# Scores of two heads interleaved on TensorE, the local mask moved to VectorE, and a periodic step table, in a kernel of attention and two MLPs

## The chip, the core and the metric

The kernel runs on one core of a Trainium2 chip. The metric is the device time of one execution in microseconds (us). The engines are TensorE (PE, with its weight loads as PEld), VectorE (DVE), ScalarE (ACT), GpSimd (POOL) and SyncE (SP), which here only issues DMAs. Each engine works through its own list in order; they meet at semaphores.

## The reference

```python
B, H, S, D = 4, 8, 576, 64;  factor = 4
# 1. attention over means of 4 tokens, repeated 4 times
q_d, k_d, v_d = means of q, k, v over groups of 4 tokens      # 144 rows
out_up = repeat(softmax(q_d @ k_d.T / 8) @ v_d, 4)
# 2. local attention: only |i - j| < 4
scores = where(|i - j| < 4, q @ k.T / 8, -1e9)
x = out_up + softmax(scores) @ v                              # 2304 x 512
# 3. first MLP
h = x @ w_in;  x = (h * cos(h)) @ w_out                       # 512 -> 2048 -> 512
# 4. second MLP: RMS norm, gate and value, silu
out = (silu(xn @ w_gate) * (xn @ w_val)) @ w_out2             # 512 -> 1536 -> 512
```

## The kernel before

**Stages.** The 32 heads are taken as 16 pairs, four per batch; a pair's two heads lie on partitions 0 to 63 and 64 to 127 of `qk`. Batch 0 is computed first, by itself, with many PSUM banks (the class `Wide`). Then the first MLP runs in six chunks of 384 tokens, and during the first three chunks the attention of batches 1, 2 and 3 is computed in the gaps (the class `Narrow`, with one bank X and one bank Z for everything). Then come three chunks without attention, and last the second MLP.

**A chunk of the first MLP.** TensorE goes through steps 0 to 18. At step f it does `up(f)` (12 matmuls of 384 columns), then what `attend(…, f, 0)` finds in its table, then the down product of f - 3 (9 matmuls of 512 columns), then what `attend(…, f, 1)` finds. Around `up(f)`, VectorE makes the angle in two instructions (L1047, L1049), ScalarE the sine (L751), VectorE the product (L1055), ScalarE the high part (L684) and VectorE the low part (L964). `up(f)` waits only for the product of f - 3. VectorE and ScalarE have the same two places per f as TensorE has, half 0 before the sine or the low part, half 1 after the product or the sine.

**A pair.** VectorE forms the means (`down_qk`). TensorE puts a mask (three bf16 matmuls against the identity) and then ten 64x64 window products into the score bank (`local`), and two products of 144 columns for the means (`downsampled`). VectorE takes the maximum and subtracts it (`less_local_max`, `down_max`), ScalarE takes the exponentials (`exps`, which needs another activation table than the sine), VectorE sums and inverts (`sum_up`), GpSimd multiplies (`normalise`), TensorE transposes (`transposes`), ScalarE and VectorE copy back, TensorE multiplies with the values (`values`), and ScalarE and VectorE add the result into the chunk's input (`copy_down`, `add_up`). In `Narrow` both heads' local scores use bank X one after the other, and both heads' mean scores bank Z.

**What sets the order.** Written tables. `PE_WHERE` gives for each of the four pairs of a batch the step and half of `scores0`, `local1`, `downsampled1`, `transposes0`, `transposes1` and `values`; `BESIDE_WHERE` does so for VectorE and ScalarE together. GpSimd has no places: it takes value sums and normalisations in order, and in the first batch also splits 16 weight units between the pairs (L517, L519).

Of the kernel before, what the change touches and what calls it, by code (L numbers as in the profile page):

```python
# [14 lines left out]
P = 128  # L15
# [32 lines left out]
WIN = 64  # L48
# [33 lines left out]
def attention_and_two_mlps(nc, qk, vwin, vgrp, w1, wgv, w2, rms_g, const, wsplit, out):  # L82
# [32 lines left out]
    identb = keep("identb", [P, P], BF16)  # L115
    maskb = keep("maskb", [P, 3, WIN], BF16)
# [38 lines left out]
    raw_const = at("raw_const", [P, P + 3 * WIN], F32, xs_at)  # L155
# [49 lines left out]
    class Narrow:  # L205
# [4 lines left out]
        sl, sd = [X[:, 0:TP * WIN]] * 2, [Z[0:QT, 0:2 * SD]] * 2  # L210
# [17 lines left out]
    down_scores = sem("down_scores")  # L228
    lmax_ready = sem("lmax_ready")
# [107 lines left out]
    def hold(eng, semaphore, value):  # L337
# [3 lines left out]
        if not isinstance(value, int):  # L341
# [5 lines left out]
    PE_STEPS = ("scores0", "local1", "downsampled1", "transposes0", "transposes1", "values")  # L347
    PE_WHERE = (((1, 0), (2, 0), (3, 0), (4, 0), (4, 1), (5, 0)),
# [3 lines left out]


    BESIDE_STEPS = ("down_qk", "less_max0", "exps", "copy_pt0", "copy_pt1", "copy_down")
    BESIDE_WHERE = (((-1, 1), (0, 0), (1, 1), (2, 1), (3, 1), (4, 1)),
# [3 lines left out]

    def steps_at(names, where, place):  # L360
        return [(name, j) for j in range(PAIRS) for name, at_ in zip(names, where[j]) if at_ == place]
# [247 lines left out]
    def act_program(act):  # L609
# [19 lines left out]
        def exps(kind, b, j, s):  # L629

            if kind is Narrow and s == 0:
# [54 lines left out]
        def attend(c, f, half):  # L686

            for what, j in steps_at(BESIDE_STEPS, BESIDE_WHERE, (f, half)):
# [170 lines left out]
    def dve_program(dve):  # L859
# [6 lines left out]
        v.tensor_copy(identb[:, :], raw_const[:, 0:P]).then_inc(setup_dve, 1)  # L866
        v.tensor_copy(maskb[:, :, :].rearrange("p a b -> p (a b)"), raw_const[:, P:P + 3 * WIN]).then_inc(setup_dve, 1)
# [23 lines left out]
        def less_local_max(kind, b, j, s):  # L891
# [3 lines left out]
            sl = kind.sl[s].rearrange("p (t k) -> p t k", k=WIN)  # L895
            dve.wait_ge(local_scores, u + 1)
            v.tensor_reduce(lmax[:, s, :], sl, axis=AX.X, op=ALU.max).then_inc(lmax_ready, 1)
            dve.wait_ge(lmax_ready, u + 1)
# [37 lines left out]

        down_qk(Wide, 0, 0)
# [28 lines left out]
        def attend(c, f, half):  # L966

            for what, j in steps_at(BESIDE_STEPS, BESIDE_WHERE, (f, half)):
                if what == "down_qk":
                    down_qk(Narrow, c + 1, j)  # L970
                elif what == "less_max0":
                    less_max(Narrow, c + 1, j, 0)
                elif what == "exps":
                    less_local_max(Narrow, c + 1, j, 1)
                    sum_up(Narrow, c + 1, j, 0)
                    down_max(Narrow, c + 1, j, 1)
# [5 lines left out]
                elif what == "copy_down":  # L982
# [180 lines left out]
    def pe_program(pe):  # L1163
        t_ = nc.tensor

        def local(kind, b, j, s):
# [3 lines left out]
            q, k = (kind.qk[j][64 * s:64 * s + 64, a, :] for a in range(2))  # L1170
            if kind is Narrow:
                if s == 0:
                    pe.wait_ge(x_ready, n)
                else:
# [328 lines left out]
```

## Time and profile before

| | |
|---|---|
| median of three runs | 973.09 us (971.92 to 973.64) |
| the profiled execution's own time | 974.04 us |
| its span | 972.3 us |
| TensorE busy | 951.9 us, 98% |
| VectorE busy | 591.2 us, 61% |
| ScalarE, GpSimd busy | 411.0 us (42%), 308.9 us (32%) |
| second chunk, from the first up matmul to that of the next chunk | 152.66 to 246.19, 93.53 us |
| in it, busy TensorE, VectorE, ScalarE, GpSimd | 93.03, 68.73, 47.40, 26.12 us |

The busy figures are averages over stages with different limits: batch 0 (up to about 55 us) is not bound by TensorE, the rest is. The third chunk takes 93.8 us (246.19 to 340.00). In a timeline, a row merges equal instructions (x20); two matmul records stand for one float32 matmul of the attention.

### The profile page before, as it was taken

The numbers are of one execution on the slowest core, as the hardware profiler recorded it, in microseconds if no ns is written. First come the engines' busy times: TensorE is split into PE (matmuls) and PEld (weight loads), VectorE is DVE, ScalarE is ACT, GpSimd is POOL, SyncE is SP. The second block draws the span as 40 slices with busy tenths as digits, with TensorE's granted clock in tenths as the row PEclk, the third lists the DMA queues.
The fourth block names the chain that finished last, engine by engine and source line by source line (L and its number), as shares of the span: only waits on it lengthen the run. The fifth ranks groups of instructions, "written<-read, shape, count | busy, mean of one in ns | idle before, by whom it ended". The sixth has DMA issues, their size and how long they took to land.

```text
span 972.3 us, 17493 instructions
## 1 busy us (share of the span) xinstructions
PE 951.9 (98%) x6104; PEld 848.5 (87%) x6104; DVE 591.2 (61%) x1225; ACT 411.0 (42%) x889; POOL 308.9 (32%) x366
## 2 busy tenths in 40 slices
PE   7899999999999999999999999999999999999998
PEld 5678888888888899999989988899899899999997
DVE  6668777776876675675768554445644456544344
ACT  4435445544644454454544433334422234433232
POOL 5948873221422165486474220011200002000000
PEclk9999999999999999999999999999999999999999
DMA  9622211111111134354345665555565555575631
GB/s 290 219 71 99 79 54 54 54 53 54 53 55 53 50 128 150 130 195 169 140 161 185 261 210 148 152 157 159 146 217 151 152 161 162 154 227 162 163 98 65
DMA packets 66173, 132.31 MB, mean 136 GB/s; under 512 B 7088, under 2 KB 7216, under 8 KB 66096
## 3 DMA queue, kind: packets, MB, share of 16 engines
q1 hardware_dynamic: 66096, 131.27, 42.8%
q8 instruction: 50, 0.82, 0.3%
q14 instruction: 27, 0.22, 0.1%
HBM read 104.50 MB, written 26.74 MB: 135 GB/s over the span
## 4 chain that ended last, share of the span: by engine, by line
PE 91%; POOL 3%; DVE 2%; issue 1%; ACT 1%; DMA 1%; SPq 0%; POOLq 0%; ACTq 0%; DVEq 0%
PE ps L1268 28%; PE ps L1270 27%; PE ps L1269 27%; POOL W L519 2%; PE ps L1187 1%; PE ps L1204 1%; PE ps L1342 1%; PE ps L1245 1%; PE ps L1221 1%; PE ps L1237 1%; DMA qk<-qk 1%; PE ps L1224 1%; DVE xs L960 0%; POOL vg_more L493 0%; POOL prob L505 0%
## 5 line engine op out<-in xcount | busy, mean ns | idle before, releaser
L1268 PE MATMUL ps<-xo,wu 128*128 128x384 f32 x504 | 168.7, 335 | 1.5 <-DVE gate_a L1090 1.5
L1269 PE MATMUL ps<-xo,wu 128*128 128x384 f32 x504 | 169.9, 337 | 0.0
L1270 PE MATMUL ps<-xo,wu 128*128 128x384 f32 x504 | 169.4, 336 | 0.0
L1268 PE MATMUL ps<-xs,W 128*128 128x384 f32 x384 | 134.6, 350 | 0.9 <-DVE xs L960 0.9
L1270 PE MATMUL ps<-xs,W 128*128 128x384 f32 x384 | 130.5, 340 | 0.0
L1269 PE MATMUL ps<-xs,W 128*128 128x384 f32 x384 | 130.1, 339 | 0.0
L1268 PE MATMUL ps<-W,ring 128*128 128x512 f32 x288 | 116.4, 404 | 0.1
L1270 PE MATMUL ps<-W,ring 128*128 128x512 f32 x288 | 113.4, 394 | 0.0
L1269 PE MATMUL ps<-W,ring 128*128 128x512 f32 x288 | 113.2, 393 | 0.0
L751 ACT ACTIVATE ub<-ub,consts 128x384 f32<-128x384 f32 x96 | 59.1, 616 | 104.9 <-DVE ub L1049 104.2
L1268 PEld LDWEIGHTS ps<-xo,wu 128*128 128x128 f32 x504 | 94.7, 188 | 8.2 <-DVE gate_a L1090 1.8
L1269 PEld LDWEIGHTS ps<-xo,wu 128*128 128x128 f32 x504 | 94.6, 188 | 6.7
L1270 PEld LDWEIGHTS ps<-xo,wu 128*128 128x128 f32 x504 | 94.7, 188 | 0.0
L1270 PE MATMUL ps<-wo,ring 128*128 128x512 f32 x216 | 85.7, 397 | 0.0
L1269 PE MATMUL ps<-wo,ring 128*128 128x512 f32 x216 | 85.4, 395 | 0.0
L1268 PE MATMUL ps<-wo,ring 128*128 128x512 f32 x216 | 85.3, 395 | 0.1
L1047 DVE TENSOR_SCALAR ub<-ps 128x384 f32<-128x384 f32 x96 | 53.0, 552 | 49.3 <-PE ps L1270 49.2
L1095 DVE TENSOR_TENSOR val_b<-val_b,ps 128x384 f32<-128x384 f32 x36 | 20.0, 555 | 98.8 <-ACT val_b L798 98.7
L1268 PEld LDWEIGHTS ps<-xs,W 128*128 128x128 f32 x384 | 73.1, 190 | 6.3 <-issue 1.7
L1269 PEld LDWEIGHTS ps<-xs,W 128*128 128x128 f32 x384 | 73.2, 191 | 1.9
L964 DVE TENSOR_TENSOR ring<-ub,ring 128x384 fp32r<-128x384 f32 x96 | 67.1, 699 | 10.9 <-ACT ring L684 10.6
L1270 PEld LDWEIGHTS ps<-xs,W 128*128 128x128 f32 x384 | 73.1, 190 | 0.0
(132 smaller groups left out, 1730.4 us busy)
## 6 DMA issues: line engine op xcount, KB each, us to landing
wu<-wsplit SPq DMA_DIRECT2D x252, 256.0 KB, 2.8
wsplit<-wp SPq DMA_DIRECT2D x84, 256.0 KB, 2.0
W_raw<-w SPq DMA_DIRECT2D x8, 1024.0 KB, 14.6
qk<-qk SPq DMA_DIRECT2D x14, 576.0 KB, 4.2
gv<-wgv SPq DMA_DIRECT2D x12, 512.0 KB, 3.7
vw<-vwin SPq DMA_DIRECT2D x14, 384.0 KB, 3.2
out<-XY SPq DMA_DIRECT2D x18, 256.0 KB, 3.6
vg<-vgrp SPq DMA_DIRECT2D x26, 144.0 KB
```

What stands on the lines that cost most here:

```text
L519: g.tensor_tensor(lo, raw, hi.bitcast(F32), ALU.subtract).then_inc(unit_ready, 1)
L751: a.activation(v, v, ACT.Sin, scale=-2.0 * math.pi, bias=consts[:, 1:2]).then_inc(cos_ready, 1)
L964: v.tensor_tensor(ring[:, f % 3, 1, :], ub[:, f % 2, :], ring[:, f % 3, 0, :].bitcast(F32), ALU.subtract).then_inc(glo_ready, 1)
L1047: v.tensor_scalar(w, HB[f % NH], 0.25, MAGIC, ALU.add, ALU.add).then_inc(angle0, 1)
L1095: v.tensor_tensor(vb[:, :], vb[:, :], CB, ALU.add).then_inc(vb_ready, 1)
L1187: ins = t_.matmul(sl[64 * half:64 * half + 64, t * WIN:t * WIN + WIN], q[:, Q0[w]:Q0[w] + WIN], k[:, K0[w]:K0[w] + WIN], start=False, stop ...
L1204: ins = t_.matmul(kind.sd[s][:, t * SD:t * SD + SD], q[:, t * QT:t * QT + QT], k, start=True, stop=True)
L1221: t_.transpose(kind.pt[:, k * P:k * P + P], kind.prob[j][:, s, 2 * k:2 * k + 2, :].rearrange("p a b -> p (a b)"), ident[:, :])
L1224: ins = t_.transpose(kind.ptd[:, k * SD + t * QT:k * SD + t * QT + QT], kind.probd[j][0:QT, s, t, k * QT:k * QT + QT], ident[0:QT, 0:QT])
L1268: t_.matmul(dst, a_lo, b_hi, start=first, stop=False, skip_group_check=True)
L1269: t_.matmul(dst, a_hi, b_lo, start=False, stop=False, skip_group_check=True)
L1270: return t_.matmul(dst, a_hi, b_hi, start=False, stop=last, skip_group_check=True)
```

## The change

Three things change together. The mask is no longer accumulated by TensorE: it is stored for all five tiles (`maskb` of 5 x 64 columns, `identb` goes, and the constant that is loaded grows from 320 to 448 columns), and VectorE adds it in an instruction of its own. In the chunks, both heads' scores are computed side by side, alternating head by head, one head in bank X and the other in bank Z (local scores X and Z, mean scores the same two once the masked sums are out). And the tables become one row that repeats every four steps from step 4j + 1 for pair j: TensorE's `local` at 0, `downsampled` at 1, `transposes0` at 2 (half 1), `transposes1` at 3, `values` at 3 (half 1). The means are formed two steps ahead. VectorE and ScalarE have tables of their own.

```diff
-    PE_STEPS = ("scores0", "local1", "downsampled1", "transposes0", "transposes1", "values")
-    PE_WHERE = (((1, 0), (2, 0), (3, 0), (4, 0), (4, 1), (5, 0)),
...
+    PE_STEPS = ("local", "downsampled", "transposes0", "transposes1", "values")
+    PE_AT = ((0, 0), (1, 0), (2, 1), (3, 0), (3, 1))
+    DVE_STEPS = ("down_qk", "diff", "down_max", "sum0", "sum1", "copy_pt0", "copy_pt1", "add_up")
+    DVE_AT = ((-2, 1), (0, 0), (1, 0), (1, 1), (2, 0), (2, 1), (3, 0), (3, 1))
+    ACT_STEPS = ("exps", "copy_pt0", "copy_pt1", "copy_down")
+    ACT_AT = ((1, 1), (2, 1), (3, 0), (3, 1))
...
             dve.wait_ge(local_scores, u + 1)
-            v.tensor_reduce(lmax[:, s, :], sl, axis=AX.X, op=ALU.max).then_inc(lmax_ready, 1)
-            dve.wait_ge(lmax_ready, u + 1)
             free = n - kind.lag
             if not (isinstance(free, int) and free < 0):
                 dve.wait_ge(pv_done, free + 1)
-
+            v.tensor_tensor(p, sl, maskb[:, :, :], ALU.add).then_inc(masked_ready, 1)
             v.memset(kind.prob[j][:, s, TP, :], 0.0)
-            v.tensor_tensor(kind.prob[j][:, s, 0:TP, :], sl, lmax[:, s, :].unsqueeze(2).to_broadcast([P, TP, WIN]), ALU.subtract).then_inc(diff_ready, 1)
+            dve.wait_ge(masked_ready, u + 1)
+            v.tensor_reduce(lmax[:, s, :], p, axis=AX.X, op=ALU.max).then_inc(lmax_ready, 1)
+            dve.wait_ge(lmax_ready, u + 1)
+            v.tensor_tensor(p, p, lmax[:, s, :].unsqueeze(2).to_broadcast([P, TP, WIN]), ALU.subtract).then_inc(diff_ready, 1)
...
-            t_.matmul(sl[:, 0:WIN], identb[:, :], maskb[:, 0, :], start=True, stop=False, skip_group_check=True)
...
+        def local_both(kind, b, j):
+
+            n = PAIRS * b + j
+            pe.wait_ge(x_ready, n)
+            pe.wait_ge(kind.qk_in[j], 16 * loads(kind, b, j))
+            for w in range(NW):
+                for s in range(2):
+                    ins = local_window(kind, j, s, w)
+            ins.then_inc(local_scores, 2)
+
+        def downsampled_both(kind, b, j):
+
+            n = PAIRS * b + j
+            pe.wait_ge(qkd_ready, n + 1)
+            pe.wait_ge(masked_ready, 2 * n + 2)
+            for t in range(2):
+                for s in range(2):
+                    ins = downsampled_tile(kind, j, s, t)
+            ins.then_inc(down_scores, 2)
```

VectorE, the first pair of a chunk, from the chunk's first product (L1055) to the inverse of the first head's sums. `ub` is the angle and then the product, `ring` the low part, `prob` the local scores of the pair. Before:

```order
L1055 SCALAR_TENSOR_TENSOR ub<-ps,ub 128x384
L1047 TENSOR_SCALAR ub<-ps 128x384
L1049 SCALAR_TENSOR_TENSOR ub<-ub,ps 128x384
L964 TENSOR_TENSOR ring<-ub,ring 128x384
L1055 SCALAR_TENSOR_TENSOR ub<-ps,ub 128x384
L897 TENSOR_REDUCE lmax<-ps 128x5
L903 MEMSET prob_81 128x64
L904 TENSOR_TENSOR prob_81<-ps,lmax 128x320
L923 TENSOR_REDUCE sums<-prob_81 128x5
L926 TENSOR_SCALAR sums<-sums 128x7
L930 RECIPROCAL recip<-sums 128x7
```

After the change (its line numbers are those of the changed file: L894 is the new addition, L1054 the product, L960 the low part, L905 the maximum of the mean scores):

```order
L1054 SCALAR_TENSOR_TENSOR ub<-ps,ub 128x384
L1046 TENSOR_SCALAR ub<-ps 128x384
L1048 SCALAR_TENSOR_TENSOR ub<-ub,ps 128x384
L894 TENSOR_TENSOR prob_80<-ps,maskb 128x320
L895 MEMSET prob_80 128x64
L897 TENSOR_REDUCE lmax<-prob_80 128x5
L899 TENSOR_TENSOR prob_80<-prob_80,lmax 128x320
L894 TENSOR_TENSOR prob_80<-ps,maskb 128x320
L895 MEMSET prob_80 128x64
L897 TENSOR_REDUCE lmax<-prob_80 128x5
L899 TENSOR_TENSOR prob_80<-prob_80,lmax 128x320
L960 TENSOR_TENSOR ring<-ub,ring 128x384
```

The first head's maximum and difference stood ahead of the first product at f = 0, and one head's sums followed in f = 1; now both heads' additions, maxima and differences stand together in f = 1, and the sums come one step later.

TensorE, the second head of a chunk's first pair, before (a float32 row counts one per matmul, not per record):

```order
L1181 MATMUL ps<-maskb,identb 128x64
L1182 MATMUL ps<-maskb,identb 128x192
L1184 MATMUL ps<-maskb,identb 128x64
L1187 MATMUL ps<-qk_77 64x64 x10
L1268 MATMUL ps<-xs,W_49 128x384
```

After, in place of two such groups and of two groups of L1204 with x2, each pair has these two rows, an `up` apart, and its transposes stand half a step behind the third `up`:

```order
L1169 MATMUL ps<-qk_76 64x64 x20
...
L1175 MATMUL ps<-qkd_82 72x144 x4
...
L1226 MATMUL ps<-ident,prob_80 128x128 x3
L1229 MATMUL ps<-ident,probd_81 72x72 x4
```

Three insertions of scores per pair have become two, and no mask stands among them.

## Rows read from the trace of the kernel before

**Rows 1.** The page: busy time of each engine, its share of the span.

```profile
PE 951.9 (98%) x6104; PEld 848.5 (87%) x6104; DVE 591.2 (61%) x1225; ACT 411.0 (42%) x889; POOL 308.9 (32%) x366
```

**Rows 2.** Timeline of PE: start, duration, engine, line, operation, tiles, records.

```profile
203.54 0.20 PE L1181 MATMUL ps<-maskb,identb 128*128 128x64 bf16 x1
...
203.78 0.80 PE L1187 MATMUL ps<-qk 64*64 64x64 f32 x20
204.51 0.45 PE L1268 MATMUL ps<-xs,W 128*128 128x384 f32 x1
204.80 0.34 PE L1269 MATMUL ps<-xs,W 128*128 128x384 f32 x1
204.97 0.35 PE L1270 MATMUL ps<-xs,W 128*128 128x384 f32 x1
...
206.56 0.34 PE L1270 MATMUL ps<-xs,W 128*128 128x384 f32 x1
206.82 0.71 PE L1204 MATMUL ps<-qkd 64*72 64x144 f32 x4
207.46 0.50 PE L1268 MATMUL ps<-W,ring 128*128 128x512 f32 x1
207.80 0.39 PE L1269 MATMUL ps<-W,ring 128*128 128x512 f32 x1
208.03 0.39 PE L1270 MATMUL ps<-W,ring 128*128 128x512 f32 x1
```

**Rows 3.** Timeline of PE, the products with the values of one pair.

```profile
146.96 0.71 PE L1237 MATMUL ps<-probd,vd 72*64 72x144 f32 x8
147.60 0.91 PE L1245 MATMUL ps<-prob,vw 64*64 64x58 f32 x40
```

**Rows 4.** Timeline, start of the second chunk: PE's first up, then DVE.

```profile
152.66 0.33 PE L1268 MATMUL ps<-xs,W 128*128 128x384 f32 x1
...
157.05 0.55 DVE L1047 TENSOR_SCALAR ub<-ps 128x384 f32<-128x384 f32 x1
157.63 0.55 DVE L1049 SCALAR_TENSOR_TENSOR ub<-ub,ps 128x384 f32<-128x384 f32 x1
158.10 0.49 DVE L897 TENSOR_REDUCE lmax<-ps 128x5 f32<-128x320 f32 x1
...
158.70 0.43 DVE L904 TENSOR_TENSOR prob<-ps,lmax 128x320 f32<-128x320 f32 x1
159.04 0.44 DVE L910 TENSOR_REDUCE dmax<-ps 72x2 f32<-72x288 f32 x1
```

**Rows 5.** Timeline: ACT's sine and table load, then POOL's end of a normalisation.

```profile
161.68 0.62 ACT L751 ACTIVATE ub<-ub,consts 128x384 f32<-128x384 f32 x1 [0.53 <-DVE ub L1049]
162.31 1.28 ACT L624 ACT_TABLE_LOAD   x1
...
166.93 0.66 POOL L508 TENSOR_TENSOR probd<-probd,recip 72x288 f32<-72x288 f32 x1 [0.18 <-POOL prob L505]
```

**Rows 6.** Groups of instructions by line on PE: busy, mean ns, idle before.

```profile
L1204 PE MATMUL ps<-qkd 64*72 64x144 f32 x128 | 26.8, 338 | 0.8 <-ACT probd L624 0.8
```

**Rows 7.** Timeline of POOL in the first chunk.

```profile
75.96 1.24 POOL L517 TENSOR_TENSOR W<-W_raw,ones 128x512 fp32r<-128x512 f32 x1
...
89.17 0.72 POOL L493 TENSOR_TENSOR vg<-vg 72x256 f32<-72x256 f32 x1
...
94.31 0.72 POOL L505 TENSOR_TENSOR prob<-prob,recip 128x320 f32<-128x320 f32 x1
```

**Rows 8.** Timeline of POOL in batch 0: two of its normalisations.

```profile
15.01 0.72 POOL L505 TENSOR_TENSOR prob<-prob,recip 128x320 f32<-128x320 f32 x1 [1.54 <-DVE recip L930]
...
47.66 0.66 POOL L508 TENSOR_TENSOR probd<-probd,recip 72x288 f32<-72x288 f32 x1
```

**Rows 9.** Timeline of DVE in the first chunk, while POOL splits weights.

```profile
85.55 1.27 DVE L964 TENSOR_TENSOR ring<-ub,ring 128x384 fp32r<-128x384 f32 x1
```

**Rows 10.** DMA issues of the page: KB of each, median us to landing.

```profile
qk<-qk SPq DMA_DIRECT2D x14, 576.0 KB, 4.2
```

More of the change, by code:

```diff
@@ L342, in hold @@
             eng.sem_inc(passed, 1)
-    PE_STEPS = ("scores0", "local1", "downsampled1", "transposes0", "transposes1", "values")
-    PE_WHERE = (((1, 0), (2, 0), (3, 0), (4, 0), (4, 1), (5, 0)),
[3 rows of a table removed]
-    BESIDE_STEPS = ("down_qk", "less_max0", "exps", "copy_pt0", "copy_pt1", "copy_down")
-    BESIDE_WHERE = (((-1, 1), (0, 0), (1, 1), (2, 1), (3, 1), (4, 1)),
[3 rows of a table removed]
+    PE_STEPS = ("local", "downsampled", "transposes0", "transposes1", "values")
[4 more added lines that the diff above has]
+    ACT_AT = ((1, 1), (2, 1), (3, 0), (3, 1))
     def steps_at(names, where, place):
-        return [(name, j) for j in range(PAIRS) for name, at_ in zip(names, where[j]) if at_ == place]
+        return [(name, j) for j in range(PAIRS) for name, (step, half) in zip(names, where) if (4 * j + 1 + step, half) == place]
     def x_arrived(eng, c, k):
@@ L686, in attend @@
         def attend(c, f, half):
-            for what, j in steps_at(BESIDE_STEPS, BESIDE_WHERE, (f, half)):
+            for what, j in steps_at(ACT_STEPS, ACT_AT, (f, half)):
                 if what == "exps":
@@ L1164, in pe_program, with local_window, downsampled_tile @@
         t_ = nc.tensor
-        def local(kind, b, j, s):
+        def local_window(kind, j, s, w):
+            q, k = (kind.qk[j][64 * s:64 * s + 64, a, :] for a in range(2))
+            half, t = w % 2, w // 2
+            return t_.matmul(kind.sl[s][64 * half:64 * half + 64, t * WIN:t * WIN + WIN], q[:, Q0[w]:Q0[w] + WIN], k[:, K0[w]:K0[w] + WIN],
+                             start=True, stop=True)
+        def downsampled_tile(kind, j, s, t):
+            q, k = (kind.qkd[j][64 * s:64 * s + 64, a, :] for a in range(2))
+            return t_.matmul(kind.sd[s][:, t * SD:t * SD + SD], q[:, t * QT:t * QT + QT], k, start=True, stop=True)
@@ L1168, in local, with scores @@
+        def scores(kind, b, j, s):
             n = PAIRS * b + j
             u = 2 * n + s
[L1170 to L1174, printed above, removed]
-                    pe.wait_ge(diff_ready, u)
-            elif u > 1:
-                pe.wait_ge(diff_ready, u - 1)
+            if u > 1:
+                pe.wait_ge(masked_ready, u - 1)
             if s == 0:
@@ L1196, in downsampled @@
                 pe.wait_ge(qkd_ready, n + 1)
-            if kind is Narrow:
-                if s == 1:
-                    pe.wait_ge(exp_down, u)
-            elif u > 1:
+            if u > 1:
                 pe.wait_ge(exp_down, u - 1)
-            q, k = (kind.qkd[j][64 * s:64 * s + 64, a, :] for a in range(2))
             for t in range(2):
-                ins = t_.matmul(kind.sd[s][:, t * SD:t * SD + SD], q[:, t * QT:t * QT + QT], k, start=True, stop=True)
+                ins = downsampled_tile(kind, j, s, t)
@@ L1291, in attend @@
         def attend(b, step, half):
-            for what, j in steps_at(PE_STEPS, PE_WHERE, (step, half)):
-                if what == "scores0":
-                    scores(Narrow, b, j, 0)
-                elif what == "local1":
-                    local(Narrow, b, j, 1)
-                elif what == "downsampled1":
-                    downsampled(Narrow, b, j, 1)
+            for what, j in steps_at(PE_STEPS, PE_AT, (step, half)):
+                if what == "local":
+                    local_both(Narrow, b, j)
+                elif what == "downsampled":
+                    downsampled_both(Narrow, b, j)
                 elif what == "transposes0":
```

57 lines of the change are left out of this document (25 added, 32 removed), and 6 rows, old and new, of tables (BESIDE_WHERE, PE_WHERE).

## The prediction

> **What bounds the kernel now.** I read the page first. TensorE is busy in 98% of the span, VectorE in 61% [rows 1]. Then the timelines of the chunks with attention: there TensorE's matmuls follow one another, and its only idle time that the grouped view puts down to another engine in the attention's score matmuls is 0.8 us in all, before the mean scores [rows 6]. So from the first chunk on, TensorE time taken out is time gained, as long as nobody else gets late. The other engines are late by little: in a chunk's first pair VectorE takes up its first angle only 4.39 us after TensorE's first up matmul (157.05 against 152.66) [rows 4]. Batch 0, ahead of the chunks, is another stage: from 15 us to 48 us GpSimd works almost without a break, with normalisations at both ends [rows 8].
>
> **What TensorE saves.** A full-size matmul starts 0.17 (384 columns) or 0.23 us (512) after the one before it; an up is 12 x 0.175 = 2.10, a down 9 x 0.23 = 2.07. The second head's masks and windows cost 204.80 - 203.54 - 0.17 = 1.09: 0.24 of masks, 0.73 of windows, 0.12 of return to full size. Its mean scores cost 207.80 - 206.56 - 0.17 - 0.23 = 0.84, of which 0.09 is the way into the small tiles. The first head has both in one insertion, 1.09 + 0.64 = 1.73 [rows 2]. Sum for a pair: 3.66.
>
> How much two heads side by side cost isn't in the trace, so I bound it. Window products with 20 records take 0.80, the value products with 40 records, which alternate in both halves of the array's rows and columns, 0.91; the mean scores take 0.71 for 4 records in whole-width tiles one after the other, the mean's values 0.71 for 8 records that alternate between two column halves [rows 2, 3]. So one bound is "two heads for the price of one", the other "no overlap". I take the first, since the value rows are the nearest. Then a pair costs 0.09 + 0.73 + 0.12 = 0.94 for windows and 0.84 for means, 1.78 together, and 3.66 - 1.78 = 1.88 is saved. Times 12 pairs: **-22.6 us**. Without overlap 0.6 + 0.5 = 1.1 us per pair are missing from it, 13 us in all.
>
> **What arrives late instead: a chunk's first pair.** I write the step times down from the first up matmul (0). TensorE: up(0) and up(1) to 4.2, windows to 5.14, up(2) to 7.24; there it wants the mean scores, which now wait for both heads' masked sums, since they go into the same banks. VectorE starts its first angle at 4.39, the second instruction 0.58 later, and ScalarE's sine follows 0.59 behind that. A VectorE instruction of this size gives way to an independent one after 0.47; a maximum of 320 columns and the subtraction behind it take 0.60 and 0.34 [rows 4]. f = 0: angle 4.39 and 4.97, sine 5.56, product 6.20. f = 1: angle 6.68 and 7.26, first addition 7.73. The addition has no row of its own; the nearest is the subtraction of the same 320 columns out of PSUM, 0.43 [rows 4], and 0.08 to the instruction that needs it. So addition, maximum, subtraction are 0.51 + 0.57 + 0.34 = 1.42 per head, the second addition starts at 9.15 and is done at 9.6. TensorE has waited **2.4 us**.
>
> From there VectorE goes on: maximum and subtraction of the second head to 10.57, low part and product to 11.5, angle of f = 2 at 11.5 and 12.1, sine at 12.7. From a sine to the end of the first head's normalisation the trace has 161.68 to 167.59, 5.91 us, of which 1.28 is the load of the exponential's table [rows 5]. So the transposes can begin at 18.6. TensorE, from 9.6, has mean scores, up(3), down(0) to do, 0.84 + 2.10 + 2.07, and stands at 14.6: **4.0 us** of hole. Before, the first transposes stood behind up(4), and each head's scores went their own way.
>
> The first chunk starts with TensorE slow (below), and VectorE is not behind there; only the second hole counts, with 0.15 of the first. Sum over three chunks: 2 x 6.4 + 4.15 = 16.9, less the 0.8 that stood there before: **+16.1**.
>
> **The other nine first transposes.** Counted from the third up's end, TensorE comes to them after 0.84 + 2.07 + 2.10 + 2.07 = 7.08. VectorE sees that end 0.2 late, needs 0.58 + 0.59 for the angle, and the chain of 5.91 follows: 7.28, plus 0.05 of semaphore: a hole of 0.25 for six pairs, 1.5 us. In the first chunk GpSimd splits five units behind each pair: 75.96 to 89.17 is 13.2, to the next normalisation 5.1 more [rows 7]; with two normalisations of 1.5 (0.72, 0.66 and their gaps) [rows 5, 7] is 21.3, and it begins about 0.6 after the transposes; a pair's four steps take TensorE 4 x 4.17 + 1.78 + 2.9 (transposes, values) = 21.4. Hole about 0.6 with the semaphore, three times: 1.8. Together **+3.3**.
>
> **The last pair's second transposes** stand directly behind the first, without a product between (there is no up(16)). GpSimd normalises the second head 0.5 behind the first, 1.5 long; TensorE is there after 0.63. Hole 1.35, three times: **+4.0**.
>
> **Batch 0.** Masks leave TensorE there too, but GpSimd sets the pace, and what counts is when its row of work starts. Both additions of the first pair lie ahead of it. The first is covered by the wait for the second pair's load; the second is not: +0.5. The subtraction now reads SBUF twice, as L964 does, which took 1.27 while GpSimd worked, where others of 384 columns take 0.55 [rows 4, 9]: 0 to 0.7 more. The constant's load grows by 64 KB ahead of the first `qk`, 0.2 to 0.5 when 576 KB take 4.2 [rows 10]. **+1.1**, between 0.6 and 1.5. The later pairs have more room than they lose.
>
> That a subtraction with two SBUF inputs waits for GpSimd is also what the Trainium skill says (SBUF — State Buffer, "Who interferes with whom": a VectorE instruction with two SBUF inputs contends with a GpSimd instruction that reads SBUF). By a reading in which GpSimd never matters, the sum would be 0.6 lower; the row decides for the rule.
>
> **Nothing for** the means two steps ahead (that step of VectorE holds only an angle, a product and copies besides, and the `qk` load, 4.2 us [rows 10], has a step and a half), the memset, the shorter setup. If that cover were gone, the mean's 1.3 us would stand in front of an angle, and the chain behind would be late by as much.
>
> **Sum.** -22.6 + 16.1 + 3.3 + 4.0 + 1.1 = +1.9. The profiled execution took 974.04, so 975.9 on its scale. The median of the runs lies 0.95 lower, so I say 975.0. Its own range is 972 to 979: the chain enters 12 holes, so 0.2 us less in it are 2.4 us less in all, and a lock of 0.3 per pair is 3.6 more. VectorE has no cover for such a lock: in the step with both heads' masks it works 0.58 + 0.47 + 2 x 1.42 + 0.95 = 4.84, and TensorE ends the next up 0.94 + 2.07 + 2.10 = 5.11 after the last. A measurement here tells about 0.2% (1.95 us) from nothing.
>
> **Rivals.**
> (a) *The holes are smaller than I make them, and the kernel is faster.* The point is the chain behind a chunk's first pair. If half of the 16.1 goes, the result is 967; if all 23.4 stayed out, 952. For it: what I chain are starts with waits in them. Against: every link is a row, and the order on VectorE and ScalarE is fixed. It decides from 4 us less hole in all on. 0.17.
> (b) *The clock falls in the holes.* The granted clock reads 1.00 throughout, but ahead of 62.8 us the same up matmuls follow one another by 0.32 instead of 0.17 us, behind a stage in which TensorE did small attention products and waited, so the lower of the levels, 1.2 GHz, exists here. A fall in a hole of 4.0 us would cost what that start costs, some 13 matmuls x 0.15 = 1.9, in each of three chunks: 981. Against: holes are short beside the busy stretches. 0.12. The Trainium skill's page TensorE: Matmul & The Clock Gate, Part 1, says that an array left idle goes back to half rate, and speaks against this change; its own sum would be this rival's.
> (c) *The heads don't overlap.* 13 us are missing, but a TensorE that is slower also waits less (each transposes' hole shrinks by what stands ahead of it, about 5 us in all): 983. Against it stand the value rows. 0.08.
> (d) *My sum*, 0.63, about a third of it within 0.2% of before.
>
> **Numbers.** Likeliest 975.0. The range takes in (d), the nearer part of (a) and (b): 969 to 982. Faster by over 0.2% is (a) with a rest of (d): 0.18. Within: 0.27. Slower: (b), (c) and the rest of (d): 0.55.
>
> **What would show it.** Right: no L1181 to L1184; 40 window records in 0.8 to 0.9 us; TensorE idle about 2.4 us before the mean scores and 4 us before the transposes of each first pair in the second and third chunk, with GpSimd's normalisation as releaser; a chunk about as long as before (93.5 us). Wrong: a chunk of 88 us or less (then the chain was shorter), 40 records in 1.5 us (no overlap), or up matmuls 0.32 us apart behind a hole (the clock).

## The result, and the profile after

| | before | after |
|---|---|---|
| median of 4 runs each | 973.37 us | 987.82 us (986.53 to 991.8) |
| ratio, 95% interval | | 1.0162 (1.0145 to 1.018) |
| span of the profiled execution | 972.3 us | 984.7 us |
| start of the first, second, third, fourth chunk | 54.96, 152.66, 246.19, 339.54 us | 56.98, 157.43, 254.77, 352.00 us |

The change makes the kernel 1.6% slower. I had forecast 975.0 us within 969 to 982: the sign was right, the time is 12.8 us off and outside my range. Behind the start of the fourth chunk the two executions are the same again; the 12.4 us between the spans arise before. (The third chunk of the kernel before ends at 339.54 us, so it took 93.35 us, not the 93.8 given ahead.) One execution of `before_shifted` below took 1316.6 us at a mean granted clock of 0.67, a slow state, and enters no comparison.

The page of after: the busy line (it answers to [rows 1]), the instruction queues, the chain that ended last. PE is busy 16 us less in a longer span.

```profile
PE 936.1 (95%) x6008; PEld 835.0 (85%) x6008; DVE 603.8 (61%) x1256; ACT 409.7 (42%) x889; POOL 310.5 (32%) x366
...
q14 instruction: 38, 0.31, 0.1%
...
PE 77%; DVE 10%; issue 6%; ACT 4%; POOL 2%; DMA 0%; DVEq 0%; ACTq 0%; SPq 0%; POOLq 0%
```

The windows of after, one row a chunk with attention; behind the busy times of the engines stands the granted clock:

```profile
56.98:157.43 100.45, 91.35 (x779) 77.39 (x777) 75.84 (x189) 45.96 (x100) 61.34 (x64) 0.97 0.22 73
157.43:254.77 97.34, 89.28 (x777) 76.08 (x776) 72.24 (x183) 46.84 (x104) 25.11 (x37) 0.96 0.18 54
254.77:352.00 97.23, 88.57 (x777) 75.39 (x776) 72.05 (x183) 46.84 (x104) 25.35 (x37) 0.96 0.16 50
```

The second chunk took 93.53 us before. TensorE now has 89.28 us of work in it instead of 93.03 and is 3.8 us slower through it: 8 us of holes (stretches in which TensorE waits), and a clock that reads 1.00 no longer.

PE's timeline at the second chunk's first pair (the place of [rows 2]):

```profile
161.71 0.81 PE L1169 MATMUL ps<-qk 64*64 64x64 f32 x40
162.45 0.44 PE L1273 MATMUL ps<-xs,W 128*128 128x384 f32 x1
...
169.95 1.24 PE L1175 MATMUL ps<-qkd 64*72 64x144 f32 x8 [5.15 <-DVE prob L894]
171.12 0.69 PE L1273 MATMUL ps<-xs,W 128*128 128x384 f32 x1
171.61 0.52 PE L1274 MATMUL ps<-xs,W 128*128 128x384 f32 x1
171.93 0.52 PE L1275 MATMUL ps<-xs,W 128*128 128x384 f32 x1
...
178.84 0.55 PE L1226 MATMUL ps<-ident,prob 128*128 128x128 f32 x3 [1.15 <-POOL probd L502]
```

Three readings. The 40 windows take 162.45 - 161.71 = 0.74 us: the heads overlap. The mean scores wait 5.15 us, where I had 2.4. And behind that wait the same up matmuls follow one another by 0.32 instead of 0.17 us. The windows of the same stretch show the granted clock (the third number from the end) fall to 0.50, which is 1.2 of 2.4 GHz, within the 5 us without a matmul:

```profile
162.00:166.00 4.00, 2.81 (x48) 2.42 (x40) 2.37 (x3) 0.30 (x1) 3.34 (x5) 1.00 0.01 2
166.00:170.00 4.00, 0.05 (x2) 0.08 (x3) 3.59 (x10) 1.45 (x3) 1.23 (x2) 0.87 0.48 135
170.00:174.00 4.00, 4.00 (x17) 3.63 (x18) 3.86 (x11) 1.63 (x3) 0.00 (x0) 0.50 0.37 99
174.00:178.00 4.00, 3.70 (x14) 2.89 (x12) 2.67 (x7) 3.97 (x13) 0.72 (x1) 0.78 0.23 85
```

Why 5.15? VectorE's timeline at the start of the same chunk (the place of [rows 4]):

```profile
158.46 2.13 DVE L1067 COPY XY<-ps 128x512 f32 x3 [1.67 <-ACT ub L768]
163.26 1.35 DVE L869 TENSOR_REDUCE qkd<-qk 128x288 f32<-128x1152 f32 x1 [2.67 <-issue]
164.53 0.55 DVE L1046 TENSOR_SCALAR ub<-ps 128x384 f32<-128x384 f32 x1
```

Between the last instruction of the loop over the chunks (L1067) and its first (L869) VectorE stands still for 2.67 us and waits for nothing that the profile names ("issue"). The first angle comes 7.10 us after the first up, not 4.39 [rows 4]. In the full list of VectorE's instructions the next one comes 3.02 and 2.93 us after the compare-and-branch that jumps back; before the change it was 0.31 and 0.28 (measured from start to start). The page's q14 row (instruction packets, 8 KB each) has 38 packets where the page of before has 27.

### The profile page after: what moved, and what is told of

The parts are those of the page before. It is cut to its first block, busy times and chain, and to the rows that moved or that the text cites. A ratio compares the mean times of both kernels' runs of the same rounds, so it can differ in the third digit from the quotient of the medians.

```text
span 984.7 us, 17345 instructions
## 1 busy us (share of the span) xinstructions
PE 936.1 (95%) x6008; PEld 835.0 (85%) x6008; DVE 603.8 (61%) x1256; ACT 409.7 (42%) x889; POOL 310.5 (32%) x366
## 4 chain that ended last, share of the span: by engine, by line
PE 77%; DVE 10%; issue 6%; ACT 4%; POOL 2%; DMA 0%; DVEq 0%; ACTq 0%; SPq 0%; POOLq 0%
PE ps L1273 24%; PE ps L1275 23%; PE ps L1274 23%; DVE ub L1046 2%; ACT L618 2%; PE ps L1250 1%; PE ps L1226 1%; DVE prob L894 1%; PE ps L1242 1%; DVE lmax L897 1%; PE ps L1345 1%; DVE ub L1048 1%; POOL prob L499 1%; ACT probd L618 1%; DVE ring L960 1%
## 5 line engine op out<-in xcount | busy, mean ns | idle before, releaser
L960 DVE TENSOR_TENSOR ring<-ub,ring 128x384 fp32r<-128x384 f32 x96 | 65.1, 678 | 9.5 <-ACT ring L678 9.5
```

Source lines behind the costliest of these rows:

```text
L960: v.tensor_tensor(ring[:, f % 3, 1, :], ub[:, f % 2, :], ring[:, f % 3, 0, :].bitcast(F32), ALU.subtract).then_inc(glo_ready, 1)
```

## The experiments

**Is the pause a load of code?** Counted in the traces from 0, VectorE's loop body ran from its instruction 139 to 443 before and from 147 to 459 after (eight additions a chunk). The Trainium skill, Advanced Engine Details and Errata, "ISA Cache", says that an engine holds code in two lines of 256 instructions. By that, a body that touches a third line can't stay resident. I had not weighed that rule. The next two kernels move the body and change no work, by one edit that stands ahead of everything (56 in after_shifted, 16 in before_shifted):

```diff
         v = nc.vector
+        for n in range(56):
+            v.memset(X[:, n:n + 1], 0.0)
         v.memset(consts[:, 0:1], MAGIC).then_inc(zeroed, 1)
```

after_shifted. 

> The changed kernel with 56 one-column memsets on VectorE ahead of everything (they write scratch columns of PSUM that nobody reads, at a time when VectorE waits for a constant). They only shift the later code of VectorE by 56 instructions. Theory (instruction fetch): the 2.9 us between the jump back at the end of VectorE's loop over the chunks and its next instruction are a load of code, which depends on how many blocks the loop body touches; the body (313 instructions in the trace) starts at the 147th instruction and ends at the 459th, and if blocks are 128 instructions with a border near 450 it touches four of them; shifted by 56 it touches three. Then the jump takes 0.3 us as before the change, the hole ahead of the first mean scores falls from 5.2 to about 2.6 us in the second and third chunk, and the time falls by at least 5.2 us to 982.6; to 978 if the clock then stays up too. Rival (the pause is a wait of the new order, not a fetch): no change, 987.8.

Measured: 982.86 us, ratio to before 1.0102 (1.0084 to 1.012). The body stands at 203 to 515. Page and timeline:

```profile
q14 instruction: 28, 0.23, 0.1%
```

```profile
158.87 2.13 DVE L1069 COPY XY<-ps 128x512 f32 x3 [1.67 <-ACT ub L768]
161.00 1.35 DVE L871 TENSOR_REDUCE qkd<-qk 128x288 f32<-128x1152 f32 x1
```

No pause, and the time is the 982.6 expected; the wait of the mean scores is 2.48 us, my 2.4. From 159 to 164 us, around the jump, q14 moved one packet here and three in the kernel after the change.

before_shifted. 

> The kernel before with 16 such memsets on VectorE, nothing else. Theory (fetch): its loop body (305 instructions, from the 139th to the 443rd) now ends at the 459th and touches a fourth block; the jump back takes about 3 us instead of 0.3, twice; VectorE's first product is 2.7 us later, and TensorE, which had about 1 us to spare there, waits 1.5 to 2 us per chunk: 976 to 977.5 instead of 973.4. Rival (the pause belongs to the new order): 973.4, jump of 0.3.

Measured: 978.04 us, 1.0052 (1.0034 to 1.007), body at 155 to 459; the second and third chunk take 95.88 and 95.81 us instead of 93.53 and 93.35.

```profile
q14 instruction: 38, 0.31, 0.1%
```

```profile
152.15 2.13 DVE L1070 COPY XY<-ps 128x512 f32 x3 [1.68 <-ACT ub L774]
156.78 1.35 DVE L878 TENSOR_REDUCE qkd<-qk 128x288 f32<-128x1152 f32 x1 [2.49 <-issue]
```

Its time is 0.5 us above the 976 to 977.5 expected; its pauses are 2.85 and 2.79 us, and TensorE waits 1.83 and 1.76 us behind them. So the load of code (the "fetch" of the expectations) holds on both sides: the same work gets the pause or loses it when the body is moved. The pause doesn't belong to the new order. A border lies between the instructions 444 and 459; the kernel before ended at most 15 short of it. How long the blocks of code are is not settled: three blocks of 128, as my expectation had it, fit all these runs as well as two of 256.

**Which part of the change costs?**

masks_only (the addition alone, in the kernel before):

```diff
+            v.tensor_tensor(p, sl, maskb[:, :, :], ALU.add).then_inc(masked_ready, 1)
...
-                    pe.wait_ge(diff_ready, u)
+                    pe.wait_ge(masked_ready, u)
...
-            t_.matmul(sl[:, 0:WIN], identb[:, :], maskb[:, 0, :], start=True, stop=False, skip_group_check=True)
```

> The kernel before (its tables, its scores head by head) with the mask added by VectorE alone. TensorE saves 24 x 0.24 = 5.8 us of mask matmuls. Batch 0 costs 2.0 more (as measured in the changed kernel). Theory (fetch): eight additions lengthen the loop body to 313 instructions as in the changed kernel, so the jump pause of 3 us is there as well and costs 1.5 to 2 us twice: about 973. Rival (the pause comes from the new order): no pause, 969.6. If the additions themselves make VectorE late in the first pair, 1 us per chunk more in either case.

Measured: 978.33 us, 1.0053 (1.0035 to 1.0071). The pause is there (2.87 and 2.79 us; body again 147 to 459, 38 packets), and behind it 2.0 us of idle TensorE and up matmuls 0.32 us apart. The pause was predicted; the time is 5.3 us above the 973 expected, and the next kernel shows that most of this is neither pause nor clock.

masks_only_shifted (the same with the 56 memsets). 

> masks_only with 56 memsets ahead, so that the loop body of VectorE no longer touches a further block. masks_only measured 978.3: chunks of 95.7 us with a pause of 2.9 us at the jump, 2 us of TensorE idle before the first mean scores and a granted clock of 0.98. Theory (pause plus the clock's fall are what it costs; the additions themselves are hidden): the hole and the fall go, each of the second and third chunk gets 2.2 + 1.3 us shorter, to 92.2; 978.3 - 7 = 971 to 972, slightly under the kernel before, since TensorE saves 5.8 us and batch 0 costs 2.5. Rival (the additions themselves make VectorE late): 974 to 976.

Measured: 974.42 us, 1.0013 (1.0003 to 1.0022): 3.9 us less than masks_only, the pause gone and the clock at 1.00, but not the 971 to 972 of the theory; it is the rival's 974 to 976 (the additions make VectorE late). TensorE still waits 1.05 and 1.43 us before the mean scores of the first pairs, and the first chunk begins at 58.16 us, 3.2 later than before. So what the masks save on TensorE (5.8 us) is spent on VectorE's later chain and in batch 0.

interleave_only (the new order, masks left on TensorE: the diff of the change without its lines on `maskb` and `masked_ready`). 

> The changed kernel (both heads side by side, new table) with the masks still accumulated by TensorE and no addition on VectorE. TensorE has 12 x 0.48 = 5.8 us more. VectorE's chain to the second head's release of its bank is as long (maximum, difference, maximum, difference), behind it 0.9 us shorter. The loop body is back at 305 instructions. Theory (fetch): no pause at the jump; hole ahead of the first mean scores 1.9 us, ahead of the first transposes about 2.6; the 0.32 us holes of the later pairs vanish; batch 0 as before: 981 if the clock falls behind the holes as in the changed kernel, 976 if it stays up. Rival (the pause comes from the new order): 5 to 6 us more than that.

Measured: 977.87 us, 1.0043 (1.003 to 1.0057); body 139 to 443, no pause, as expected. The waits of the second chunk's first pair:

```profile
161.43 0.71 PE L1180 MATMUL ps<-qkd 64*72 64x144 f32 x8 [2.14 <-DVE prob L898]
...
169.26 0.55 PE L1234 MATMUL ps<-ident,prob 128*128 128x128 f32 x3 [2.73 <-POOL probd L502]
```

So the order alone costs its first pair's two holes, and each half of the change by itself is no faster than before. The half that crosses the border is the masks.

The halves don't add up. With the pause gone from both, the masks cost 0.13%, the order 0.43%, and the two together (after_shifted) 1.02%. The starts of the chunks say where: the first begins at 54.75 us in interleave_only and at 57.73 in after_shifted, the second at 151.59 and 157.84, and behind that after_shifted is the faster one (190.62 us against 191.75 for two chunks). So the additions cost 2 to 3 us in batch 0 (the kernel after the change, without memsets ahead, begins its first chunk at 56.98) and 3.3 in the first chunk, the two stretches in which GpSimd also splits weights. Under the old order they cost as much in batch 0 (57.43 in masks_only) but nothing in the first chunk, which takes 95.00 us there.

**What does the clock cost?** fill_holes:

```diff
+    FILL = {"downsampled": 12, "transposes0": 14}
...
+                if j == 0 and what in FILL:
+                    pe.wait_ge(g_done, F1 * (b - 1) + step + 2)
+                    for _ in range(FILL[what]):
+                        t_.matmul(HB[(step + 1) % NH], w_part(2 * step, 0)[:, 0:P], xs[:, 0, 0, :], start=True, stop=True, skip_group_check=True)
```

> after_shifted with matmuls whose results nobody reads, put into a chunk's two first-pair waits of TensorE: 12 of 384 columns before the first mean scores, 14 before the first transposes (they write the bank of the next up matmul, which overwrites it). The computation is as before. TensorE waits as long as before but is busy meanwhile. Theory (the granted clock falls because TensorE was idle, and costs 1 to 2 us after each hole): no stretch of the attention chunks is granted less than 0.9; the second and third chunk get 1.5 to 2 us shorter, the first loses 1.3 us more than it gains in the first hole (12 x 0.17 = 2.1 us in a hole of 0.8) and gains 1.4 behind the second: 979 to 980 against the 982.9 of after_shifted. Rival (the clock falls for another reason, for instance power or the small score matmuls): clock as in after_shifted, 983 to 984.

Measured: 983.15 us, 1.0096 (1.008 to 1.0113): nothing gained, where I had expected 979 to 980. Behind the filled holes the matmuls keep their distance of 0.17 us, but the time goes into the next wait (the first transposes stand until GpSimd has normalised, whether TensorE was slow before or not), and the clock now fell at the last pairs of the first and second chunk.

fill_all (the waits over 0.5 us of those chunks filled in this way). 

> after_shifted with matmuls whose results nobody reads in every wait of TensorE over 0.5 us of the attention chunks: before the first mean scores 4 in the first chunk and 15 in the other two, before the first transposes 22 and 20, before those of pairs 2 and 3 a few (3 and 9 in the first chunk, 1 later), between the last pair's transposes 7. The computation is as before. Theory (the clock falls behind idle time, and costs real time only where nothing later is waited for anyway): the falls of after_shifted that count are those behind the first chunk's first transposes (1.5), its third pair (1.35) and the second chunk's last pair (1.5), 4.4 us together: no stretch under 0.95, 978 to 979. Rival (the rest of the difference is holes, the clock costs nothing net): 982.9, or some tenths more for fillings that are too long.

Measured: 981.13 us, 1.0092 (1.0075 to 1.0109). Its windows, a row a chunk:

```profile
57.85:157.50 99.65, 96.35 (x824) 83.47 (x822) 76.25 (x189) 45.87 (x100) 61.64 (x64) 1.00 0.22 74
157.50:252.07 94.57, 94.21 (x821) 81.32 (x820) 71.67 (x183) 46.84 (x104) 25.77 (x37) 1.00 0.18 55
252.07:346.47 94.40, 94.06 (x822) 81.25 (x821) 71.77 (x183) 46.83 (x104) 25.43 (x37) 1.00 0.17 51
```

and those of after_shifted:

```profile
57.73:157.84 100.11, 91.26 (x778) 77.81 (x777) 75.32 (x189) 45.94 (x100) 61.51 (x64) 0.97 0.22 73
157.84:254.00 96.16, 89.81 (x777) 76.31 (x776) 71.88 (x183) 46.84 (x104) 25.47 (x37) 0.96 0.17 54
254.00:348.46 94.46, 88.18 (x777) 75.23 (x776) 71.77 (x183) 46.83 (x104) 25.34 (x37) 0.98 0.17 51
```

The clock stays at 1.00, though three holes of 0.7 to 1.3 us are left in the first chunk: with TensorE busy in the others the falls are gone, so they come from idleness. What they cost is small and depends on the place. The third chunk of after_shifted had a clock of 0.98 and is as long as with 1.00, because its fall lay ahead of a hole. The second had one more, behind the last pair's transposes, where nothing waits afterwards: nine down matmuls took 3.81 us there instead of 2.24, and the chunk is 96.16 instead of 94.46. The gain of 1.7 us in the medians is within the two intervals, so only the traces show it; the 4.4 us that I expected did not come.

**Can the holes be taken out?** pairwise:

```diff
+            for s in range(2):
+                sl = kind.sl[s].rearrange("p (t k) -> p t k", k=WIN)
+                v.tensor_tensor(kind.prob[j][:, s, 0:TP, :], sl, maskb[:, :, :], ALU.add).then_inc(masked_ready, 1)
...
+            v.tensor_reduce(lmax[:, :, :], p, axis=AX.X, op=ALU.max).then_inc(lmax_ready, 2)
...
+            v.tensor_tensor(p, p, lmax[:, :, :].unsqueeze(3).to_broadcast([P, 2, TP, WIN]), ALU.subtract).then_inc(diff_ready, 2)
```

> after_shifted, VectorE takes both heads of a pair together in the chunks: both additions first, then one maximum and one subtraction over both heads (640 columns). The second bank is released after two additions (1.0 us) instead of addition, maximum, subtraction, addition (1.93), and the whole takes about 2.45 instead of 2.9. Theory (the hole ahead of the first mean scores is VectorE's chain up to the second addition): that hole falls from 2.7 to 1.8, the one ahead of the transposes by another 0.4, and the 0.3 us holes of the later pairs by 0.2 to 0.3: 3 x 1.9 - 0.5 = about -5 us, 978; if the clock stays up then, 975. Rival (the holes come from something later, the table load or GpSimd): 982.9.

Measured: 986.18 us, 1.013 (1.0113 to 1.0147), *slower* than after_shifted (1.0102) by some 3 us. Its trace is of the slowest of its four executions (988.75 us):

```profile
165.88 0.71 PE L1192 MATMUL ps<-qkd 64*72 64x144 f32 x8 [1.43 <-DVE prob L910]
...
175.57 0.69 PE L1243 MATMUL ps<-ident,prob 128*128 128x128 f32 x2 [4.61 <-POOL probd L502]
```

The first hole shrank from 2.48 to 1.43 as expected. But VectorE's chain as a whole is only 0.25 us shorter (both heads in 2.65 instead of 2.90), so the time went into the next hole (2.23 to 4.61; between the two holes TensorE needed 5.08 us instead of 6.66, since no slow clock fell there, and that too is waited for). And behind this single long one the clock fell where it counts: the up behind it took 3.99 us instead of 2.17. The expectation added up holes of which the second is the first one's remainder.

own_first_row and own_row_pairwise give the first pair its own places:

```diff
+    PE_FIRST = ((0, 0), (1, 0), (3, 0), (3, 1), (4, 0))
+    DVE_FIRST = ((-2, 1), (-1, 1), (0, 0), (0, 1), (1, 0), (1, 1), (2, 0), (3, 0))
+    ACT_FIRST = ((0, 1), (1, 1), (2, 0), (3, 0))
```

> after_shifted with a row of its own for each batch's first pair: VectorE adds, takes maxima and subtracts after the first product (f = 0, half 1) instead of ahead of the second, ScalarE takes the exponentials and VectorE the rest one half step or more earlier than the periodic row says, and TensorE comes to the first transposes half a step later (after the fourth up), to the second after the next down, and to the values after the fifth up. Theory (the loss is the VectorE chain behind a chunk's first pair): the addition of the second head ends 1.1 us earlier (hole 1.6), the exponentials come a whole step earlier, so no hole ahead of the transposes: per chunk -1.1, -2.9 (-3.8 in the first) and with them most of the clock's fall (-1.7): about 982.9 - 17 = 966, 3 us more if the product of f = 1, which is now late by 2.8 us, makes an up wait. Rival (the gaps only move to the next place, the values or the second pair's scores): 978 or more.

> Both of the last two edits together. If they add up: own_first_row minus 3 to 4 us (the first hole falls to 0.6, three small holes of later pairs by 0.2 to 0.3 each in three chunks), so about 962 to 963. Rival (once the first pair is in order nothing waits for VectorE's chain): the time of own_first_row.

Measured: 978.54 us, 1.0051 (1.0034 to 1.0068), and 976.68 us, 1.0046 (1.0031 to 1.006). Chunks of 94.42 and 92.87, and of 93.99 and 92.11 us. Against after_shifted that is 4.3 us where some 17 were expected (the time is the rival's, 978 or more), and 6.2 where some 20 were. The trace of the second shows holes that are left or new: in each of these chunks 1.7 us between the first pair's values and the second's windows (VectorE has to empty the banks), and 2.05 and 1.44 us before the first down (the profile names no releaser; in VectorE's order the low part of f = 0 stands behind the mean maxima).

own_row_mended moves these places (OWN1 is the second pair), the next two build on it:

```diff
-    DVE_FIRST = ((-2, 1), (-1, 1), (0, 0), (0, 1), (1, 0), (1, 1), (2, 0), (3, 0))
+    DVE_FIRST = ((-1, 0), (-1, 1), (0, 1), (0, 1), (1, 0), (1, 1), (2, 0), (3, 0))
+    OWN1 = {PE_AT: ((0, 1), (1, 0), (2, 1), (3, 0), (3, 1)), DVE_AT: DVE_AT, ACT_AT: ACT_AT}
```

> own_row_pairwise with three places moved, each after a wait that its trace shows. (1) The second pair's windows go behind the next down product instead of directly behind the first pair's values: TensorE waited 1.75 us there for VectorE to empty the banks. (2) The first pair's mean maxima stand behind the product of f = 1 instead of ahead of the low part of f = 0: the first down waited 1.6 us for that low part. (3) The means of the first pair are formed after the chunk's first angle instead of ahead of it (1.27 us of VectorE at the chunk's start, 0.69 of it now beside the sine). Theory (in the attention chunks all that is left to gain is waits for VectorE's order): each chunk 3 to 3.5 us shorter, about 89 in the second and third, and hardly a hole in which the clock could fall: 976.7 - 10 to 12 = 965 to 967. Rival (each wait taken away appears at the next place, as in pairwise): 973 or more.

> own_row_mended, with the masks of batch 0 alone back on TensorE (they are multiplied with every second bf16 half of the float32 identity, and VectorE takes maximum and difference from PSUM there as before). Theory (batch 0 is bound by VectorE and GpSimd, not by TensorE, and VectorE's additions and the longer constant cost 2 to 2.7 us there): the first chunk begins at about 55.2 instead of 57.7, the rest is the same: 2.5 us faster than own_row_mended, about 963. Rival (batch 0 is late for another reason, e.g. the code or the load of the constant): no change.

> masks_in_batch0_on_pe, with the last pair's second transposes of TensorE behind the next down product and its values behind the one after. Theory (the hole of 1.33 us between the last pair's transposes is the wait for the second normalisation): it goes, but the values come 0.7 to 2 us later with one down product (2.04 us) instead of two behind them, and copying, adding and splitting take about 2.5 us until the next chunk's first up: from 1 us faster to 2 us slower in all; likeliest within 1 us. Rival (the split isn't ready in time): 1 to 1.5 us per chunk slower.

Measured: 975.32 us, 1.0026 (1.0015 to 1.0038); 977.33 us, 1.0037 (1.0023 to 1.0051); 970.2 us, 0.9972 (0.9957 to 0.9988). The first was a miss (965 to 967 expected, its rival 973 or more), for a reason that its trace gives: the second pair's windows now come half a step later and its transposes didn't, so they wait 1.82 us, with a clock's fall behind them. (That trace is of its slowest execution, 980.42 us; the other seven lie between 974.89 and 976.84.) The masks of batch 0 back on TensorE let the first chunk begin at 56.0 and 55.2 us (the traces of the second and third kernel) instead of 57.5, but no gain shows in the medians (the second kernel's is even 2.0 us higher; its runs lie between 971.9 and 978.27). Spreading the last pair is the first version under the kernel before. It gained 7.1 us where at most 1 was expected: the three holes of 1.3 us between the last pair's transposes are gone, 3.9 us, and its trace has two falls of the clock instead of four; how much of the rest these account for was not tried.

half_step_rows carries that on to every pair. It still has the joint subtraction of pairwise, the masks of batch 0 on TensorE and the idle memsets ahead:

```diff
+    PE_HALF = ((0, 1), (1, 0), (3, 0), (3, 1), (4, 0))
+    PE_LAST = ((0, 1), (1, 0), (2, 1), (3, 1), (4, 1))
...
+            rows = (PE_FIRST, PE_HALF, PE_HALF, PE_LAST)
```

> last_pair_spread, and now every pair but the first has its windows behind the down product (half 1) and every pair but the last its first transposes behind the next up instead of ahead of it, the second behind the down product after it and the values behind the up after that, so that no two steps of a pair stand side by side. VectorE's and ScalarE's tables are as before. In last_pair_spread TensorE waits 2.0 us before the second pair's first transposes in each chunk, and the clock falls behind it (1.5 us). Theory (the waits are differences of a few us between VectorE's chain and TensorE's distance, and a step more of distance takes them away): the hole of the second pair goes, with it the fall; chunks of 88 to 88.5 us instead of 90 to 91.4, 970.2 - 3 x 2.5 = about 962.5. Rival (VectorE, which waits in its order for the later transposes and values, now makes an up late): no gain or a loss, 970 or more.

> half_step_rows, with the first pair's mean maxima on VectorE between the low part of f = 0 and the product of f = 1, where VectorE waits 0.7 us for the sine, instead of behind that product. The hole before the first pair's first transposes was 1.15 us. Theory: that chain is 0.5 to 0.6 us earlier, the hole 0.6: 1.5 us faster than half_step_rows. Rival (the hole is set by the sine and the exponentials of ScalarE, which come in the same order): no difference.

Measured: 966.21 us, 0.9937 (0.992 to 0.9953), and 966.73 us, 0.9941 (0.9925 to 0.9958). half_step_rows is 0.6% faster than the kernel before. Its windows:

```profile
55.19:155.64 100.45, 91.98 (x778) 77.33 (x777) 74.29 (x180) 45.80 (x100) 62.75 (x65) 0.98 0.22 73
155.64:244.81 89.17, 86.79 (x777) 73.80 (x777) 70.17 (x176) 46.58 (x105) 25.08 (x37) 1.00 0.19 59
244.81:333.71 88.90, 86.52 (x778) 73.81 (x777) 70.15 (x176) 46.61 (x105) 25.35 (x37) 1.00 0.16 50
```

The second and third chunk lose 4.4 us each against before. The first does not (100.45 us against 97.70), and there lies most of the 3.7 us by which the expectation was missed; this trace is of the slowest of four executions (968.35 us, the others 965.43 to 966.23). Moving the mean maxima did nothing: the first pair's hole stays at 1.0 us.

## Why the prediction was wrong

Between the profiled spans 12.4 us were measured and 1.9 predicted. That the sign came out right is mostly luck: 10.5 of the 12.4 us are not in my sum. By its own steps (a hole is counted here to the next start that was possible, which is 0.15 to 0.2 us more than the bracket of the timeline for the transposes):

- *What TensorE saves (-22.6).* Right: 0.74 us for 40 windows and 0.64 for the eight mean scores, to the next start. "The heads don't overlap" is out.
- *"VectorE starts its first angle at 4.39".* This is the step that failed. I took the start of the chunk over from the trace of before, as if only instructions could move it. It is 7.10, because the longer code no longer stays loaded across the jump back. The same chain from there is right: with the pause gone the hole is 2.48 for my 2.4, and from the sine to the end of the normalisation it is 5.91 us in both. Price: 2.7 us in two chunks, 5.4, half of the 10.5; the shift gave back 5.0 in the medians.
- *Rival (b), the clock.* It came true in all three chunks, with 0.12 on it. Its size was wrong in both directions: in the second and third chunk the fall behind 5.2 us of idleness lengthened TensorE's work (in the second by 2.7 us) and cost nothing, since the transposes behind it waited for the chain anyway (their hole is 1.3 and 2.2, where I had 4.0); in the first chunk it counts twice, 1.1 + 0.4 behind the first transposes and 1.4 at the last pair, together 3.0.
- *The other first transposes (+3.3).* In the later chunks 0.30 to 0.34 for my 0.25 (no row showed the 0.2 and 0.05 us that I added there for seeing an end and for a semaphore). In the first chunk 0.6, 1.9 and 1.5 for my 0.6 each, 2.2 more. GpSimd's queue, on which I had put it, was not behind (it waited for VectorE's inverse, 1.65, 1.04 and 0.72 us). VectorE was slow itself beside GpSimd's splitting; the new subtraction and the low part, which both read SBUF twice:

```profile
110.54 1.43 DVE L899 TENSOR_TENSOR prob<-prob,lmax 128x320 f32<-128x320 f32 x1
...
112.93 0.49 DVE L899 TENSOR_TENSOR prob<-prob,lmax 128x320 f32<-128x320 f32 x1
113.34 1.63 DVE L960 TENSOR_TENSOR ring<-ub,ring 128x384 fp32r<-128x384 f32 x1
```

  GpSimd beside it:

```profile
110.33 1.29 POOL L513 TENSOR_TENSOR W<-W_raw,W 128x512 fp32r<-128x512 f32 x1
...
112.95 1.60 POOL L513 TENSOR_TENSOR W<-W_raw,W 128x512 fp32r<-128x512 f32 x1
```

  The subtraction that starts behind GpSimd's instruction takes 1.43 us, the one that starts 0.02 ahead of it 0.49, and then GpSimd's takes 1.60 instead of about 1.28. interleave_only, whose subtraction reads PSUM, has no hole over 0.3 us before the first transposes of the other three pairs of this chunk; since it has no additions either, it doesn't tell the two apart, and the lock's share of the 2.2 us is read from the rows only.

  I knew this lock [rows 9] and priced it in batch 0 alone, and as 0.3 a pair in the range.
- *The last pair (+4.0).* 1.5 for 1.35 per chunk, right.
- *Batch 0 (+1.1).* The last split before the first chunk starts at 59.48 for 58.50, so 1.0: right. Part of it is made good because the up matmuls are at 0.17 us from 59.7 us on, not from 62.8: the second up begins only 0.5 later (60.73 for 60.24).

Sum over the measured terms beyond my 1.9: pause 5.4, clock 3.0, first chunk's holes 2.2 and 0.5 at its first pair, 1.1 of small parts in the other two chunks, less 1.7 around the start of the first chunk (0.6 in batch 0, 1.1 of slow clock that the chunk has less than before): 12.4.

My range was too narrow by construction: it treated the holes' starts as known. What made it wrong acts ahead of the chain that I had worked out so closely, and behind it.

Not settled: what the clock's falls cost on average. The kernels with holes scatter by 1 to 6 us between runs; a profile shows one execution, and in it the places of the falls differ from kernel to kernel. And how much of the first chunk's extra time in half_step_rows is VectorE's slowness beside GpSimd and how much its new table was not tried.

## What to carry to other kernels

Before adding instructions to a loop, look at where its body stands in the engine's code: here eight more carried its end over a border and cost 5 us, and 56 idle ones in front of the program gave them back. A few packets more in the page's instruction queue and an "issue" idle at the loop's first instruction are the sign.

A hole is not a price of its own: shortening the first of two that one chain governs only lengthens the second (pairwise), and a slower engine in front of a hole costs nothing as long as the hole is the longer. Add distance between a pair's steps where the chain is longest, and don't let two dependent steps stand side by side; that took the kernel from +1.0% (after_shifted) to -0.6%, with the masks of batch 0 back on TensorE, where faster instructions alone (pairwise) made it +1.3%.

## What the runs showed of the hardware

- VectorE's jump back takes 0.28 to 0.35 us with the body at 139 to 443 or 203 to 515, and 2.8 to 3.0 us at 147 to 459 or 155 to 459. This fits the two lines of 256 instructions of the Trainium skill (Advanced Engine Details and Errata, "ISA Cache"), if a border lies between 444 and 459; packets of 8 KB are what the queue shows, and no run here shows the length of a line.
- TensorE's granted clock fell to half in or behind holes of 5.15 us (after), 2.48 (after_shifted), 2.0 (masks_only) and even 1.3 (the last pair's transposes, with small products around them). It did not fall behind 1.43 us in pairwise, 1.83 in before_shifted, 2.62 in the first chunk of interleave_only and 2.86 in that of half_step_rows, and behind the same hole of 1.82 us it fell in the third chunk of last_pair_spread and not in the second. So the length of a hole by itself doesn't tell whether a fall follows. With matmuls in the holes (fill_all) it stayed at 1.00.
- A VectorE subtraction of 320 columns with both inputs in SBUF took 0.49 us alone and up to 1.43 when GpSimd's work on 512 columns had begun before it. When it began 0.02 us ahead of GpSimd it took 0.49, and GpSimd's instruction 1.60 instead of about 1.28.
